# Attention set-up before a two-layer MLP: table load, second group's queries and w_in products put in another order

## The reference

```
a = softmax(phi)                                  # over the 32 slots
k_m, v_m = a^T k, a^T v                           # per head: 32 x 64
attn = softmax(q k_m^T / 8);  x = attn v_m        # 4608 x 512 tokens
h = x @ w1_in;  g = where(h > 0, h, exp(min(h, 0)) - 1);  x = g @ w1_out
h = x @ w2_in;  g = h * clip(h + 3, 0, 6) / 6;            out = g @ w2_out
```

## Time and profile before

| | |
|---|---|
| time, median of 3 runs | 1638.16 us (1637.02 to 1641.31) |
| the profiled execution | 1637.58 us, of which 1635.8 us are the span |
| TensorE busy | 1579.6 us (97%) |
| VectorE, ScalarE, GpSimd busy | 659.4, 654.2, 132.2 us |
| chain that ended last, by engine | TensorE 57%, issue 37%, VectorE 2%, ScalarE 2%, GpSimd 1% |
| transfers | 79.50 MB, mean 49 GB/s |

### The profile page before, as it was taken

The page is one execution under the profiler, slowest core; times in us unless marked ns, Lnnn a source line. Parts: engine busy times, 40 slices in busy tenths (PEclk is TensorE's granted clock), DMA queues, the critical chain, the costliest instruction groups (busy, mean ns, idle before and its releaser), DMA issues.

```text
span 1635.8 us, 25445 instructions
## 1 busy us (share of the span) xinstructions
PE 1579.6 (97%) x9840; PEld 1364.1 (83%) x9840; DVE 659.4 (40%) x1163; ACT 654.2 (40%) x1363; POOL 132.2 (8%) x99
## 2 busy tenths in 40 slices
PE   4999999999999999999999999999999999999999
PEld 3788989879888798888998888888888888888887
DVE  4455555554555545555353232232323232323222
ACT  2565555545555455555573222222222222222222
POOL 0320000000000000000182101010101010101000
PEclk9899999999999999999999999999999999999999
DMA  9423221232212222120321010101010101010000
GB/s 246 136 42 66 52 59 42 47 68 52 59 38 52 64 55 59 38 52 17 143 79 65 0 52 0 52 0 51 0 51 0 51 0 51 0 49 2 7 19 26
DMA packets 178101, 79.50 MB, mean 49 GB/s; under 512 B 152400, under 2 KB 160592, under 8 KB 178000
## 3 DMA queue, kind: packets, MB, share of 16 engines
q1 hardware_dynamic: 168528, 76.07, 17.6%
q10 hardware_dynamic: 9472, 2.07, 0.8%
HBM read 59.24 MB, written 18.87 MB: 48 GB/s over the span
## 4 chain that ended last, share of the span: by engine, by line
PE 57%; issue 37%; DVE 2%; ACT 2%; POOL 1%; ACTq 1%; POOLq 0%; DVEq 0%
PE ps L281 18%; PE ps L283 18%; PE ps L282 18%; POOL rows L724 1%; PE ps L352 1%; DVE g L640 1%; PE ps L331 1%; ACT g_hi L503 0%; PE ps L302 0%; ACT g L501 0%; ACT g L499 0%; DVE g_lo L642 0%; ACTq L556 0%; PE ps L320 0%; ACTq L554 0%
## 5 line engine op out<-in xcount | busy, mean ns | idle before, releaser
L281 PE MATMUL ps<-g_hi,w_out_lo 128*128 128x288 f32 x1024 | 314.1, 307 | 0.9 <-POOL w_out_lo L713 0.6
L282 PE MATMUL ps<-g_lo,w_out_hi 128*128 128x288 f32 x1024 | 301.7, 295 | 0.0
L283 PE MATMUL ps<-g_hi,w_out_hi 128*128 128x288 f32 x1024 | 301.7, 295 | 0.0
L509 ACT ACTIVATE g<-ps,one_half 128x512 f32<-128x512 f32 x144 | 99.3, 690 | 465.6 <-PE ps L283 465.6
L648 DVE SCALAR_TENSOR_TENSOR g<-g,ps 128x512 f32<-128x512 f32 x144 | 99.2, 689 | 450.5 <-ACT g L509 450.5
L281 PE MATMUL ps<-x_hi,w_in_lo 128*128 128x512 f32 x576 | 224.1, 389 | 0.0
L283 PE MATMUL ps<-x_hi,w_in_hi 128*128 128x512 f32 x576 | 224.1, 389 | 0.0
L282 PE MATMUL ps<-x_lo,w_in_hi 128*128 128x512 f32 x576 | 224.1, 389 | 0.0
L281 PE MATMUL ps<-w_out_hi,g_lo 128*128 128x512 f32 x576 | 224.1, 389 | 0.0
L282 PE MATMUL ps<-w_out_lo,g_hi 128*128 128x512 f32 x576 | 224.1, 389 | 0.0
L283 PE MATMUL ps<-w_out_hi,g_hi 128*128 128x512 f32 x576 | 224.1, 389 | 0.0
(11 more groups left out here) (108 smaller groups left out, 1950.7 us busy)
## 6 DMA issues: line engine op xcount, KB each, us to landing
layer_out<-y_sb SPq DMA_DIRECT2D x16, 576.0 KB, 3.1
x_raw<-layer_out SPq DMA_DIRECT2D x9, 1024.0 KB, 6.9
kv<-in_k SPq DMA_DIRECT2D x60, 144.0 KB, 3.4
kv<-in_v SPq DMA_DIRECT2D x60, 144.0 KB, 3.5
q<-in_q SPq DMA_DIRECT2D x60, 144.0 KB, 2.9
w_in_raw<-in_moe_w_in SPq DMA_DIRECT2D x8, 1024.0 KB, 10.9
w_out_raw<-in_moe_w_out SPq DMA_DIRECT2D x8, 1024.0 KB, 6.2
out<-out_sb SPq DMA_DIRECT2D x8, 1024.0 KB, 5.1
```

What stands on the lines that cost most here:

```text
L281: nc.tensor.matmul(dst, a_lo, b_hi, start=first, stop=False)
L282: nc.tensor.matmul(dst, a_hi, b_lo, start=False, stop=False)
L283: return nc.tensor.matmul(dst, a_hi, b_hi, start=False, stop=last)
L509: nc.scalar.activation(g2[f % 2][:], hid(f, BLOCK), ACT.Relu, bias=one_half[:, 0:1], scale=1.0 / 6.0).then_inc(e_made, 1)
```

## The change

On ScalarE a one-column exponential of `one_half` (written to a tile that is not in use yet) stands between the requests for phi and those for k and v of group 1, so that the table load comes there; the requests for q of group 1 stand behind the two exponentials of phi. SyncE requests q of group 0 ahead of the first block of w_in. No item is left before the scores: items 0 and 1 stand behind them, PRE is 2, and the first half makes items 2 to 7 in its steps 0 to 5.

```diff
@@ -52,7 +52,7 @@
     LAG = 2
     RING = 4
     AHEAD = 2
-    PRE = 4
+    PRE = 2
     assert RING > LAG + 1
     assert MAC * M == P and 2 * DH == P and GROUPS == UNITS1 and H == 2 * MAC
 
@@ -246,7 +246,7 @@
 
         def items_in(u, parity):
             if isinstance(u, int) and u == 0:
-                return {0: 4, 1: 5, 2: 6, 3: 7}
+                return {0: 2, 1: 3, 2: 4, 3: 5, 4: 6, 5: 7}
             if isinstance(u, int) and u == UNITS1 - 1:
                 return {}
             return {6: 0, 7: 1, 9: 2, 10: 3, 12: 4, 13: 5} if parity else {0: 6, 1: 7}
@@ -428,11 +428,11 @@
 
             pe.wait_ge(ident_ready, 1)
             for stage in STAGES:
-                if stage in (S_SCORES, S_PT):
-                    for n in ((0, 1) if stage == S_SCORES else (2, 3)):
-                        item(n, n, n % 2, n, n)
                 attention(0, stage, A)
                 attention(1, stage, B_)
+                if stage == S_SCORES:
+                    for n in range(PRE):
+                        item(n, n, n, n, n)
             half(0, 0, True)
             half(1, 1, True)
             with pe.Fori(2, UNITS1 - 2, 4) as u:
@@ -549,18 +549,22 @@
 
             for h in range(MAC):
                 act.dma_start(B_.rows[0:ROWS, :, h * M:(h + 1) * M], phi_d[:, MAC + h]).then_inc(B_.phi_loaded, 16)
+
+            act.wait_ge(zeros_ready, 1)
+            nc.scalar.activation(g1[0][:, 0:1], one_half[:, 0:1], ACT.Exp)
             for h in range(MAC):
                 act.dma_start(B_.kv[0:ROWS, :, h, 0:DH], k_d[:, MAC + h]).then_inc(B_.kv_loaded, 16)
                 act.dma_start(B_.kv[0:ROWS, :, h, DH:2 * DH], v_d[:, MAC + h]).then_inc(B_.kv_loaded, 16)
-            for h in range(MAC):
-                act.dma_start(B_.q[h // 2][0:ROWS, :, h % 2], q_d[:, MAC + h]).then_inc(B_.q_loaded[h // 2], 16)
             for stage in STAGES:
                 if stage == S_KV:
                     act.wait_ge(zeros_ready, ZEROS)
                 attention(0, stage, A, 0)
                 attention(1, stage, B_, 1)
-                if stage in (S_Q1, S_EXP):
-                    for n in ((0, 1) if stage == S_Q1 else (2, 3)):
+                if stage == S_SUB:
+                    for h in range(MAC):
+                        act.dma_start(B_.q[h // 2][0:ROWS, :, h % 2], q_d[:, MAC + h]).then_inc(B_.q_loaded[h // 2], 16)
+                if stage == S_EXP:
+                    for n in range(PRE):
                         item(n, n, n)
             half(0, 0, True)
             half(1, 1, True)
@@ -688,8 +692,8 @@
                     dve.wait_ge(zeros_ready, ZEROS)
                 attention(0, stage, A, 0)
                 attention(1, stage, B_, 1)
-                if stage in (S_Q1, S_NORM):
-                    for n in ((0, 1) if stage == S_Q1 else (2, 3)):
+                if stage == S_NORM:
+                    for n in range(PRE):
                         item(n, n, n)
             half(0, 0, True)
             half(1, 1, True)
@@ -835,8 +839,8 @@
 
             load_phi(0, A)
             load_kv(0, A)
+            load_q(0, A)
             load_in(0, 0, w1_in_loaded[0])
-            load_q(0, A)
             load_in(1, 0, w1_in_loaded[1])
             load_out(0, 0)
             load_in(2, 0, w1_in_loaded[2])
```

## The result

| | before | after |
|---|---|---|
| median | 1638.16 us (1636.55 to 1641.31, 9 runs) | 1643.04 us (1639.49 to 1643.80, 9 runs) |
| profiled execution | 1637.58, span 1635.8 | 1643.04, span 1641.3 |
| TensorE busy | 1579.6 (97%) | 1582.9 (96%) |

The ratio is 1.0026, with a 95% interval of 1.0016 to 1.0037. The change costs 4.9 us by the two medians and 4.3 by the ratio (2.6 to 6.1), where a loss of 1.05 was forecast, and the time lies 0.7 us above the forecast's range. The interval leaves out no change: it is a small loss, but a loss.

The account below looks back on a forecast made before the run. TensorE's own work was taken to bound the dense part, and ScalarE's requests, table load and exponentials the opening. Phi's landing -0.95 and two items +2.0 gave +1.05 us, so 1639.2 us, within 1636.0 to 1642.3.

Parts of the forecast that it names:

- the phi term: First half of layer 1, step 0: row maximum starts at phi's landing, 49.2 in place of 50.17 us, winning 0.95 us.
- the items' term: Layer 1, steps 4 and 5: two items at 1.01 us each in dense TensorE work, 2.0 us paid in full.
- The front: Opening: early table load, L302 from about 17.7 us, scores earlier by 1.0 to 4.7 us, 4 taken.
- q_b did not starve: Opening: the feared case was q_b held behind w_in's packets beyond 30 us, giving +1.05 to +2.0 us; chance 0.12.
- The shift of kv_b's requests by 1.3 to 1.5 us: Opening, ScalarE: kv_b's requests move later for the table load and the one-column exponential.
- The capture of the gain by phi's landing: Step 0 of layer 1: phi lands no earlier, so VectorE waits 2 to 4 us and only 0.95 us is won.
- TensorE's wait of about 3 us: Layer 1, before the row maximum's transpose: TensorE idles about 3 us after its first two steps, then is dense.
- if that cover failed the step would wait a few tenths: Layer 1, added items: ScalarE's w_hi and VectorE's w_lo copies lie beside TensorE's work; otherwise a few tenths' wait.
- rival A: Start of the dense part: clock at half after TensorE's wait, up to 3.0 us more, +2.5 to +4.1; chance 0.22.
- the upper end of the front gain: Opening: q_b requests need not wait for the exponentials, going out a few us earlier; front gain up to 4.7 us.

Follow-up runs that it names:

- e5: Changed kernel with SyncE requesting phi of group 2 ahead of its k and v: 1637.77 us, ratio 0.9997 against the kernel before.
- e12: e5 with three unused VectorE reductions ahead of the row maximum in step 0: 1643.17 us, ratio 1.0031 against the kernel before.
- e0: The kernel before run once more, unchanged, for a second look at its transfers: 1638.47 us.
- e10: e5 with the last two items in steps 5 and 6 in place of 4 and 5: 1636.62 us, ratio 0.9985 against the kernel before.
- e11: Changed kernel with two unused fp32 products in TensorE's wait ahead of L290: 1642.47 us, ratio 1.0018 against the kernel before.
- e13: e12 with three unused fp32 products in TensorE's wait: 1645.11 us, ratio 1.0037 against the kernel before.
- e7: The changed kernel run again, unchanged: 1642.42 us, ratio 1.0019 against the kernel before.
- e9: e5 with items 2 and 3 moved into the opening, PRE 4, none in steps 4 and 5: 1636.90 us, ratio 0.9985 against the kernel before.
- e3: Changed kernel with 16 unused fp32 products in TensorE's wait ahead of L290: 1650.27 us, ratio 1.0077 against the kernel before.
- e4: Changed kernel with four unused fp32 products in TensorE's wait ahead of L290: 1643.17 us, ratio 1.0020 against the kernel before.
- e1: Kernel before with only the items moved, requests and table load as before: 1644.04 us, ratio 1.0026 against the kernel before.
- e8: Kernel before with ScalarE's part of the change and phi of group 2 requested first, items unmoved: 1639.7 us, ratio 0.9996.
- e14: Changed kernel with three unused fp32 products in TensorE's wait: 1643.48 us, ratio 1.0027 against the kernel before.
- e2: Changed kernel with the items back as before, only requests and table load changed: 1639.13 us, ratio 0.9996 against the kernel before.
- e6: Kernel before with phi of group 2 requested ahead of its k and v: 1641.23 us, ratio 1.0002 against the kernel before.

## Why the prediction was wrong

The sum had +1.05 us, and at L337 the profiled execution is 5.45 later. The 4.4 us between them are three steps: the phi term was 1.4 too low, the items' term 0.7 too low, and the half clock in the dense part, which the sum put at nothing, cost 2.3.

**Right.** The front: table load at 3.89 us, L302 held by kv's landing (at 19.0, not 17.7), scores 3.1 us earlier (4 was taken, out of 1.0 to 4.7). q_b did not starve. The shift of kv_b's requests by 1.3 to 1.5 us was wrong and did no harm: the first went out inside the table load and the last ended at 12.35, 0.64 us later than before. The capture of the gain by phi's landing: VectorE's idle time in front of the row maximum (2 to 4 us forecast, 3.69 seen), TensorE's wait of about 3 us (3.96). e5 and e12 confirm from both sides that this wait carries the loss of the front gain. The items cost their time in the dense part.

**Wrong: the phi term, -0.95.** The step that failed is "phi of group 2 lands at 49.2 as before, give or take half a us". I took one execution's landing for a constant of the program. It lies between 49.3 and 51.8 us in the seven traces with the changed order of requests, and L290 came at 52.28 and 53.26 in the two profiles of the changed kernel, +0.4 and +1.4 against 51.84. In the kernel before, a late transfer had cover: VectorE was late itself. The change took the cover away, and a late phi is now paid. That the landing was worth nothing before was in the rows; that its scatter had been hidden too was the thing to see. Whether the changed order also moves the landing by itself stays open (e0).

**Wrong: the items' term, 2.0.** It measured 2.7 at full clock (e5; 2.3 to 2.9 over the traces), of which 0.5 is the wait for w_lo in step 4. The forecast named this cover ("if that cover failed the step would wait a few tenths") and priced it at nothing. e10's trace has the 0.5 back; its median cannot show so little.

**Wrong: the choice between the forecast and rival A.** This is the largest error. The sum took TensorE to be at full clock in the dense part. The clock fell there in both profiles of the changed kernel, in e11, e12 and e13. It cost 2.3 us in the first profile, inside the 1.5 to 3.0 that A put on top of the sum, and 1.2 in e7 (41.14 us from 53.26 to 94.40, less 39.99), below it. I gave A 0.22 because two steps of unbroken work stood before the wait; the clock did come back in them (1.00 from 46.6 us), and fell again. With the sum put right it is +0.44 + 2.7 + 2.3 = 5.4. That this meets the 5.45 at L337 is no check, since 2.7 and 2.3 are the parts into which e5 divides the same difference; the checks are e9, whose stretch is back at 37.47 us without the two items, and e3 and e4, at 39.75 without the half clock. The range held A's price on top of -0.95 and 2.0, and not all three errors at once.

**Left open.** Why the fills win nothing in the median though the clock holds in the traced dense part, and why e1, without a wait for phi, loses as much as the whole change in the median. Two things in the traces may take part, but a trace exists of one execution each. One is a later fall for 3.4 us, 1.4 to 2.3 us behind L337 (88.0 to 99.2 us), in e1, e7, e8, e9, e12, e13 and e14; the other ten traces have the same wait of 1.2 us before L337 and no such fall. The other is TensorE at half speed in the opening: six query records took 1.17 us in place of 0.69 in e2, e6, e8, e13 and part of e4, and in e4 and e13 the scores were slow too. Except in e4 the clock in the profile's rows reads 1.00 there, so a mean clock near 1 does not say that TensorE was fast. Nor is it shown why the last phi piece took 4.1 us to land in e7 and 2.8 in the profile after.

## What to carry to other kernels

When a gain runs into a transfer's landing, the landing's scatter comes with it: take two or three traces of it before the sum is made, and ask which slack hid it until now. Move the transfer that is waited for first ahead of those that are not (phi ahead of k and v, worth 3.6 to 4.6 us here) before the work in front of it is made faster. An extra product in a dense stretch costs its own time and can cost a wait for the engine that finishes it (0.5 us for VectorE's w_lo here); moving the two items one step on took 0.5 of 2.7 us away.

## What the hardware showed

In four traces with a wait of 2.7 to 4.2 us ahead of L290 (after, e7, e11, e12) 6.8 us at half clock followed, beginning in the wait or up to 1.3 us behind it. In three traces with 0.46, 0 and 1.50 us of wait (e1, e5, e14) none did in the stretch, but in e13, with 1.22 us, the clock fell at 58.2 for 3.4 us, 1.9 us after L290 had started. The wait alone does not decide it, then. Four-record items on two parts of the array took 1.01 us, while the same number of records on one part took 1.9 (e11; 32 of them took 13.9 in e3). Requests that stand behind ScalarE's exponentials in the program did not wait for them: in the changed kernel the first q_b request starts at 12.46 us, while the first exponential runs from 12.40 to 13.24 and before the second starts at 13.15, and kv_b's first request starts at 3.96, inside the table load (3.89 to 5.17). So q_b went out ahead of the second exponential, as the prediction expected for the upper end of the front gain.
